# The last two experts' products as three rounded partial products instead of one full float32 product

## What is computed

```python
# attention: 2 batches, 8 heads, 768 positions, head size 64; its output x is (1536, 512)
logits = x @ w_gate                       # 1536 tokens, 8 experts
# tokens go to experts in the order of the sorted logits, 192 tokens each
for e in range(8):
    h = np.maximum(x[mask] @ w1[e], 0.0)  # 192 x 512 by 512 x 1024
    out[mask] = h @ w2[e]                 # 192 x 1024 by 1024 x 512
# dense layer on all rows
h = x @ w_in                              # 512 -> 1024
solu = h * softmax(h)
ln = (solu - mu) / np.sqrt(var + 1e-06) * g_ln
return ln @ w_out                         # 1024 -> 512
```

## Time and profile before

| | |
|---|---|
| median of 3 runs | 492.61 us |
| the profiled execution, its own time | 493.21 us |
| its span | 491.4 us (1.8 us of its time lie outside) |
| PE busy | 473.3 us, 96% of the span |
| DVE, ACT, POOL busy | 341.8, 170.8, 137.3 us |
| chain that ended last | PE 88%, DVE 5%, DMA 2% |
| mean granted TensorE clock | 0.989 of full speed |

### The profile page before, as it was taken

One profiled execution on the slowest core, in us unless ns is written; L12 is line 12 of the kernel. 1 busy time (PEld: TensorE's weight loads), 2 busy tenths in 40 slices (PEclk: granted clock), 3 DMA queues, 4 the chain that ended last, 5 costly groups with the idle time before them and its releaser, 6 DMA issues.

```text
span 491.4 us, 8510 instructions
## 1 busy us (share of the span) xinstructions
PE 473.3 (96%) x3022; PEld 414.4 (84%) x3022; DVE 341.8 (70%) x1108; ACT 170.8 (35%) x354; POOL 137.3 (28%) x213
## 2 busy tenths in 40 slices
PE   7999999999999999999999999999999999999992
PEld 5878878788889899779989988998997899899871
DVE  5777777879888998999789779968966600400451
ACT  3577778723143111433223033322302331220340
POOL 5577877520220300151131112113112141010111
PEclk9899999999999999999999999999999999999996
DMA  8987783110360540092441045045105437000001
GB/s 258 297 257 249 254 260 111 34 33 0 147 229 0 205 171 1 2 336 82 167 167 64 5 176 215 23 169 169 59 5 199 192 119 279 0 23 0 1 21 43
DMA packets 30040, 61.75 MB, mean 126 GB/s; under 512 B 6576, under 2 KB 19760, under 8 KB 25904
## 3 DMA queue, kind: packets, MB, share of 16 engines
q0 software_dynamic: 6592, 39.85, 22.0%
q1 hardware_dynamic: 22544, 20.53, 13.3%
q10 hardware_dynamic: 864, 0.84, 0.6%
HBM read 54.93 MB, written 6.29 MB: 125 GB/s over the span
## 4 chain that ended last, share of the span: by engine, by line
PE 88%; DVE 5%; DMA 2%; issue 1%; ACT 1%; SPq 0%; POOL 0%; DVEq 0%; POOLq 0%
PE psum L1157 17%; PE psum L1174 14%; PE psum L1264 6%; PE psum L1239 5%; PE psum L1246 5%; PE psum L1240 4%; PE psum L1208 4%; PE psum L945 4%; PE psum L1209 4%; PE psum L954 4%; PE psum L1218 4%; PE psum L980 4%; PE psum L977 2%; PE psum L1106 2%; PE psum L1186 2%
## 5 line engine op out<-in xcount | busy, mean ns | idle before, releaser
L1174 PE MATMUL psum<-xs,w_sb 128*128 128x192 f32 x512 | 87.0, 328 | 0.0
L1157 PE MATMUL psum<-shared,w_sb 128*128 128x192 f32 x512 | 84.6, 326 | 0.1
L1157 PEld LDWEIGHTS psum<-shared,w_sb 128*128 128x128 f32 x512 | 83.4, 190 | 1.3 <-issue 0.8
L1174 PEld LDWEIGHTS psum<-xs,w_sb 128*128 128x128 f32 x512 | 83.0, 190 | 0.0
L1546 DVE TENSOR_SCALAR_CACHE_REDUCE key_wide<-keys,thr 128x1536 bf16<-128x1536 f32 x35 | 63.3, 1808 | 0.6
L694 POOL DMA_INDIRECT w_sb<-w,widx x32 | 31.5, 984 | 95.8 <-DVE widx L1639 65.5
L718 POOL TENSOR_TENSOR gain<-spread,cst 128x1 f32<-128x1 f32 x12 | 6.8, 564 | 163.3 <-DVE spread L1701 162.4
L1668 DVE TENSOR_TENSOR yT_lo<-psum,yT_hi 128x384 fp32r<-128x384 f32 x16 | 8.8, 554 | 52.0 <-ACT yT_hi L824 51.8
L1239 PE MATMUL psum<-wout_hi,turned_hi 128*128 128x512 f32 x96 | 38.6, 402 | 1.1 <-ACT turned_hi L824 1.1
L777 ACT ACTIVATE keys<-keys,nmax 128x184 f32<-128x184 f32 x96 | 37.3, 439 | 5.3 <-DVE nmax L1378 5.3
L1208 PE MATMUL psum<-win_hi,yT_hi 128*128 128x512 f32 x96 | 38.5, 401 | 0.0
(11 more groups left out here) (186 smaller groups left out, 848.5 us busy)
## 6 DMA issues: line engine op xcount, KB each, us to landing
shared<-vT SPq DMA_DIRECT2D x8, 384.0 KB, 6.3
shared<-v_main SPq DMA_DIRECT2D x8, 384.0 KB, 3.8
x_rows<-xs SPq DMA_DIRECT2D x8, 384.0 KB, 5.0
shared<-kT SPq DMA_DIRECT2D x7, 384.0 KB, 6.6
shared<-qT SPq DMA_DIRECT2D x7, 384.0 KB, 5.6
w_sb<-w_in SPq DMA_DIRECT2D x4, 512.0 KB, 5.1
w_sb<-w_out SPq DMA_DIRECT2D x8, 256.0 KB, 5.0
w_sb<-v_tail SPq DMA_DIRECT2D x16, 48.0 KB, 3.9
```

What stands on the lines that cost most here:

```text
L1157: mm = pe.matmul(turn[u % 2][:, i * CAP:(i + 1) * CAP], w1_sb[:, par, first:first + P], xT[:, c, :], start=(c == 0), stop=(c == KC - 1))
L1174: mm = pe.matmul(turn[u % 2][:, (d % 2) * CAP:(d % 2 + 1) * CAP], w2_sb[:, par, first:first + P], hT[:, c, :], start=(c == 0), stop=(c == ...
```

## The change

For r = 6 and r = 7 every product of the expert is written as three fp32r products on the same PSUM target, each of 192 columns: high matrix by high tokens, high matrix by low tokens, low matrix by high tokens (`split_products`). The other six experts are as before.

The high part of a matrix is made by ACT as a rounding copy, the low part by DVE as a subtraction, both in four pieces of 128x1024 for each of w1 and w2 (`round_w1`, `round_w2`, `rest_of_w1`, `rest_of_w2`). The low part replaces the matrix in its own buffer, and the high part goes into the buffer of the other parity, the one of expert r - 1. Therefore the gather of w1 for r = 7 now waits for the last hidden unit of r = 6, and that of w2 for the last y of r = 6. Tokens and hidden units are stored rounded by ACT and their rests by DVE (`split_x`, `split_hidden`), in memory of the finished search. `row_numbers(7)` moves to between the hidden and the y products of r = 6; POOL gathers w2 of r = 6 ahead of its tokens; two DVE instructions at the end of the program go.

```diff
+        def rounded(name, shape):
+            return nc.alloc_sbuf_tensor_at(name, shape, F32R, offset=(nc.sbuf_base + 31) // 32 * 32)
...
+        w1_split = rounded("w1_split", [P, 2, KC * FF])
         w1_sb = sb("w1_sb", [P, 2, KC * FF])
+        w2_split = rounded("w2_split", [P, 2, FC * DM])
         w2_sb = sb("w2_sb", [P, 2, FC * DM])
...
             def gather_w1(r):
-                gather_weights(r, w1, w1_sb, in_w1)
+                gather_weights(r, w1, w1_sb, in_w1, hidden_filled[r - 1] if r - 1 in SPLIT else y_filled[r - 2])
             def gather_w2(r):
-                gather_weights(r, w2, w2_sb, in_w2)
+                gather_weights(r, w2, w2_sb, in_w2, y_filled[r - 1] if r - 1 in SPLIT else y_filled[r - 2])
...
+            def round_w1(r, pieces):
+                act.wait_ge(in_w1[r % 2], 32 * (r // 2 + 1))
+                act.wait_ge(unit_filled, hidden_filled[r - 1])
+                for j in pieces:
+                    act.activation(w1_split[:, 1 - r % 2, piece(j)], w1_sb[:, r % 2, piece(j)],
+                                   ACT.Copy).then_inc(w1_hi_ready, 1)
+            def round_w2(r, pieces):
+                act.wait_ge(in_w2[r % 2], 32 * (r // 2 + 1))
+                act.wait_ge(unit_filled, y_filled[r - 1])
+                for j in pieces:
+                    act.activation(w2_split[:, 1 - r % 2, piece(j)], w2_sb[:, r % 2, piece(j)],
+                                   ACT.Copy).then_inc(w2_hi_ready, 1)
...
+                        if ahead:
+                            round_w1(r + 1, range(2))
                         hidden_exp(n)
+                        if ahead:
+                            round_w1(r + 1, range(2, PIECES))
+                        elif r + 1 == SPLIT[0]:
+                            round_w2(r + 1, range(2, 3))
...
+            def split_products(dst, high, low, pair, first, last):
+                pe.matmul(dst, high, pair[:, 0, :], start=first, stop=False)
+                pe.matmul(dst, high, pair[:, 1, :], start=False, stop=False)
+                return pe.matmul(dst, low, pair[:, 0, :], start=False, stop=last)
+            def hidden_split(r, f):
+                par, k = r % 2, SPLIT.index(r)
+                u = at["hidden", r] + f
+                if f == 0:
+                    pe.wait_ge(x_lo_ready, 2 * k + 2)
+                unit_free(u)
+                for i in range(2):
+                    for c in range(KC):
+                        if f == i == 0:
+                            pe.wait_ge(w1_lo_ready, PIECES * k + c + 1)
+                        first = c * FF + (2 * f + i) * P
+                        mm = split_products(turn[u % 2][:, i * CAP:(i + 1) * CAP], w1_split[:, 1 - par, first:first + P],
+                                            w1_split[:, par, first:first + P], x_pair[:, c, :, :], c == 0, c == KC - 1)
+                mm.then_inc(unit_filled, 1)
+            def product_split(r, d):
+                par, k = r % 2, SPLIT.index(r)
+                u = at["y", r, d // 2]
+                if d % 2 == 0:
+                    unit_free(u)
+                for c in range(FC):
+                    if d == 0 and c % 2 == 0:
+                        pe.wait_ge(h_lo_ready, h_unit[at["hidden", r] + c // 2])
+                        pe.wait_ge(w2_lo_ready, PIECES * k + c // 2 + 1)
+                    first = c * DM + d * P
+                    mm = split_products(turn[u % 2][:, (d % 2) * CAP:(d % 2 + 1) * CAP], w2_split[:, 1 - par, first:first + P],
+                                        w2_split[:, par, first:first + P], h_pair(c), c == 0, c == FC - 1)
+                if d % 2:
+                    mm.then_inc(unit_filled, 1)
+            def split_expert(r):
+                for f in range(FC // 2):
+                    hidden_split(r, f)
+                if r == SPLIT[0]:
+                    row_numbers(r + 1)
+                for d in range(KC):
+                    product_split(r, d)
...
-                    if r + 1 == E - 2:
-                        row_numbers(E - 1)
...
+            def split_x(r):
+                for i, (first, n) in enumerate(zip(slots_of(r), (HI, LO))):
+                    u = at["tokens", r] + i
+                    dve.wait_ge(unit_emptied, u + 1)
+                    dve.tensor_tensor(x_pair[:, :, 1, first:first + n],
+                                      turn[u % 2][:, 0:KC * n].rearrange("p (c n) -> p c n", c=KC),
+                                      x_pair[:, :, 0, first:first + n].bitcast(F32), ALU.subtract).then_inc(x_lo_ready, 1)
+            def split_hidden(r, f):
+                u = at["hidden", r] + f
+                dve.wait_ge(unit_emptied, u + 1)
+                dve.scalar_tensor_tensor(h_pairs(f)[:, :, 1, :], turn[u % 2][:, 0:2 * CAP].rearrange("p (c n) -> p c n", c=2), 0.0,
+                                         h_pairs(f)[:, :, 0, :].bitcast(F32), ALU.max, ALU.subtract).then_inc(h_lo_ready, 1)
+            def rest_of_w1(r, pieces):
+                for j in pieces:
+                    dve.wait_ge(w1_hi_ready, PIECES * SPLIT.index(r) + j + 1)
+                    dve.tensor_tensor(w1_split[:, r % 2, piece(j)], w1_sb[:, r % 2, piece(j)],
+                                      w1_split[:, 1 - r % 2, piece(j)].bitcast(F32), ALU.subtract).then_inc(w1_lo_ready, 1)
+            def rest_of_w2(r, pieces):
+                for j in pieces:
+                    dve.wait_ge(w2_hi_ready, PIECES * SPLIT.index(r) + j + 1)
+                    dve.tensor_tensor(w2_split[:, r % 2, piece(j)], w2_sb[:, r % 2, piece(j)],
+                                      w2_split[:, 1 - r % 2, piece(j)].bitcast(F32), ALU.subtract).then_inc(w2_lo_ready, 1)
...
-            link(dve.tensor_scalar(key_wide[:, N // 2:N].bitcast(BF16), hits, 0.5, 0.0, ALU.is_ge, ALU.add,
-                                   accum_out=count[:, :]))
-            link(dve.tensor_scalar(hits, keys[:, :], const("cand0"), None, ALU.is_ge))
```

More of the change, by code:

```diff
@@ L419, in build, with piece @@
         y_unit = {at["y", r, d]: KC // 2 * r + d + 1 for r in range(E) for d in range(KC // 2)}
+        hidden_filled = [at["hidden", r] + FC // 2 for r in range(E)]
+        x_unit = {at["tokens", r] + i: 2 * k + i + 1 for k, r in enumerate(SPLIT) for i in range(2)}
+        h_unit = {at["hidden", r] + f: FC // 2 * k + f + 1 for k, r in enumerate(SPLIT) for f in range(FC // 2)}
+        def piece(j):
+            return slice(j * KC * FF // PIECES, (j + 1) * KC * FF // PIECES)
         norm_unit = {at["norm", n] + c: 2 * n + c + 1 for n in range(ROWS) for c in range(2)}
@@ L890, in _ @@
                 for f in range(FC // 2):
-                    empty_hidden(r, f)
+                    if r in SPLIT:
+                        empty_split_hidden(r, f)
+                    else:
+                        empty_hidden(r, f)
                     if r == 0:
                         add_flags(1, 3 + f)
+                    if r == SPLIT[0] and f == 0:
+                        round_w2(r, range(3, 4))
+                    if r == SPLIT[1] and f < 2:
+                        round_w2(r, range(2 + f, 3 + f))
                 if r == 0:
@@ L903, in _ @@
                     empty_keys(3, range(2, KEY_UNITS))
+                if r == SPLIT[0]:
+                    round_w1(r + 1, range(PIECES))
                 if r == 0:
@@ L906, in _ @@
                 for n in tiles_after(r):
+                    ahead = r + 1 == SPLIT[0] and n == tiles_after(r)[0]
                     if n >= 1:
@@ L917, in _ @@
                         hidden_squares(n)
+                    if ahead:
+                        round_w2(r + 1, range(2))
             empty_turned(ROWS - 1)
@@ new lines, in split_expert, with whole_expert @@
+            def split_expert(r):
+                for f in range(FC // 2):
+                    hidden_split(r, f)
+                if r == SPLIT[0]:
+                    row_numbers(r + 1)
+                for d in range(KC):
+                    product_split(r, d)
+            def whole_expert(r):
+                hidden(r, 0)
+                hidden(r, 1)
+                hidden(r, 2)
+                hidden(r, 3)
+                if r % 2 == 0 and r:
+                    cuts_of(r + 1)
+                product(r, 0)
+                if r % 2 == 0 and r:
+                    ranks_of(r + 1)
+                product(r, 1)
+                if r == 0:
+                    warm(WARM_CUT)
+                    cuts_of(r + 1)
+                if r % 2:
+                    cuts_of(r + 1)
+                if turns_keys(r, 1):
+                    turn_keys(r + 2)
+                product(r, 2)
+                if r % 2 or r == 0:
+                    ranks_of(r + 1)
+                product(r, 3)
@@ L1823, in _ @@
             hidden_gate(m)
+            split_x(SPLIT[0])
+            slots(E - 1)
+            slot_flags(E - 1)
             hidden_spread(m)
-            for r in (E - 2, E - 1):
+            for r in SPLIT:
+                for f in range(FC // 2):
```

(6 more changed lines are left out.)

73 lines of the change are left out of this document (45 added, 28 removed).

## The result

The changed kernel takes 494.86 us (median of 20 runs, 493.12 to 499.50), the kernel before 492.14 beside it: a ratio of 1.0054 (1.0034 to 1.0074). The same kernel run a second time gave 493.48 against 491.98, 1.0034 (1.0020 to 1.0048). So it is slower by a third to a half of a per cent, 1.5 to 2.7 us, just over what can be told from no change. The forecast was 493.8 us.

The account below looks back on a forecast made before the run. PE was taken as the bound, busy 96% of the span. Main term +1.4 us, flags -0.26 and all else hidden gave +1.15 us on the median 492.61, so 493.8 us, range 490.5 to 498.2.

Parts of the forecast that it names:

- The main term: PE, experts 6 and 7: 128 float32 products (41.6 us) become 384 fp32r products at 112 ns (43.0 us), +1.4 us.
- The rule on fast weight load: PE's weight loads: fast for 128 weights unless input is FP32; if on for fp32r, products would be bound by columns.
- Row numbers and flags: 24 small PE products move behind r = 6's hidden products, zero in all; the wait for DVE's flags goes, -0.26 us.
- ACT's pieces: 16 rounding copies at 1.05 us each, hidden ahead of empty_turned for tiles 7 and 8, slacks 0.36 and 0.7 to 1.0.
- the rival: ACT's roundings delay PE at dense_out(7) and dense_out(8): at 1.5 us a piece +1.3 us on top, 495.1 us; chance 0.12.
- DVE's pieces: 16 rests of 128x1024 on DVE at 1.15 us each, all hidden; slack 0.5 us at r = 6's last w2 piece.
- a sign of being wrong: PE waiting over 0.3 us for turned_hi, x_pair, h or w_split, or records 85 to 100 ns apart, would show error.
- The gathers: Loads of w1 and w2 for r = 7, now starting later: both hidden with 2.8 us or more.
- The sum: Whole kernel: +1.4 - 0.26 + 0 = +1.15 us, giving 493.8 us on the median of the runs.
- The columns rival: PE's split products bound by columns at 85 ns: -9.0 - 0.26, 483.3 us; chance 0.13.
- The fixed cost rival: PE's split products carry a fixed cost on top of the load, 123 ns: +5.6 - 0.26, 498.0 us; chance 0.08.
- The clock rival: Clock falls to 1.2 GHz in the split experts, products 160 ns or more: +20.6, 513 us; chance 0.05.

Follow-up runs that it names:

- the moved piece: Changed kernel with the rests of w2 in expert 7 one hidden unit earlier on DVE: 494.23 us, 1.0042 to the kernel before.
- two products: Changed kernel with high matrix by low tokens left out, 256 fp32r products instead of 384: 481.89 us.
- the wide product: Changed kernel with both products of the high matrix made one of 384 columns, halves added afterwards, rests of w2 earlier: 489.35 us, 0.9938 to the kernel before.

## Why the prediction was right, and where it was not

- **The main term** was +1.4 us at 112 ns. It measures 111.4 ns and +1.6: expert 6 +0.84 without the row numbers, expert 7 +0.76 once the wait is taken out. 384 x 0.1114 = 42.8 us are as forecast (43.0). The 0.2 comes of three small things: by PE's starts the four old blocks take 20.67 + 20.66 = 41.33 us and not 4 x 10.40 = 41.6, since the y blocks are a little shorter (10.27) than the hidden ones (+0.3); the pace is 111.4 and not 112 (-0.2); and the y block behind the row numbers takes 0.1 more. Choosing the row nearest to the case, L1239's 0.11 us at a standing start, was right, and the runs show that its reason was, too: half the columns leave 0.11 us as long as the clock is 1.00, half the load brings 90 ns.
- **The rule on fast weight load** (the Trainium skill, TensorE: Matmul & The Clock Gate, Weight-path perf modes) would have had the products bound by columns if fp32r counted as not FP32. Loads are 188 ns long after as well, as in the earlier trace rows, with 111.4 ns between them, against 104 and 32 for bf16: nothing shows it on for fp32r as it is used here, and the profile's rows name the type of these loads f32. The Trainium skill's section LDWEIGHTS on the same page gave an estimate of 107 ns and -0.6 us; the measured pace is 4 ns over it, and with the neutral point at 108 ns these few nanoseconds turn the sign.
- **Row numbers and flags**, forecast 0 and -0.26. The stretch before `hidden(6)` is 0.96 shorter where 1.03 was forecast, and the row numbers come back as 0.85. Together that is -0.11 and not -0.26: of the 0.26 us that stood idle ahead of the row numbers only a part was lost to PE. Its worth was put too low as well: putting both back costs 1.7 us, since the flags' place makes room for DVE's new pieces ahead of the gate, and the row numbers cover the last rest of w2 in expert 6.
- **ACT's pieces**, forecast 1.05 us with slacks of 0.36 and 0.7 to 1.0. Measured 0.97 to 1.06, slacks 0.52 and 1.22. Right, and the rival has no case at this place.
- **DVE's pieces**, forecast 1.15, measured 1.17 to 1.22. Here is the step that failed: "The last w2 piece of r = 6 ends at 408.1 ... Slack 0.5 us. All hidden". It was worked out for r = 6 alone. There the 0.77 us of row numbers stand between the last hidden product and the first y product. For r = 7 nothing stands there, so the same sum gives 0.5 - 0.77 = -0.3, a wait; it measured 0.61, and the moved piece takes it away exactly. The slack of 0.5 us for r = 6 was too large too: without the 0.85 us of row numbers expert 6 lost 0.52, so it was some 0.3. By the prediction's own list a wait of PE for w_split of more than 0.3 us was a sign of being wrong, and this one came.
- **The gathers** were hidden from PE, as forecast; ACT's first rounding of w1 for expert 7 (416.19) has no wait for a DMA ahead of it. For expert 6 the forecast had w1 in 0.9 us ahead of its rounding, and ACT waited 0.69 us for it (374.47), which cost PE nothing.
- **The sum**: +1.15 forecast, +1.89 by stages: +0.61 from the missed wait, +0.2 in the main term, +0.15 in row numbers and flags, and -0.2 in the stretches behind the experts, which no term had. In time it was +1.5 to +2.7. That 493.8 us lies so near the 494.86 and 493.48 is in part luck: it was added to the median of three runs, 492.61, and twenty runs of the kernel before have 492.14. The forecast put it within what can't be told from no change (0.45) and slower at 0.41; it came out slower, just over the line.
- **The columns rival** (85 ns) fell: 111.4. **The fixed cost rival** (123 ns) fell as well, and the argument against it fits: with half the load a product takes 90 ns against 80 of columns, and where the whole load is longer these 10 are not added. **The clock rival** did not come true at 192 columns (1.00 in every stretch), nor with two products; with 96 columns at the same pace it did, at the level of 1.2 GHz that it named, and a product then took 213 ns. So what this rival describes does happen here, but not with the products of this change.

What stays open: why the wide product takes 0.20 us for 384 columns (160 ns by the clock, 170 with the 10 above) while its neighbour takes 0.09. The weight loads of the same execution divide the same 0.287 us otherwise,

```profile
393.88 0.19 PEld L1310 LDWEIGHTS psum<-x_pair,w_split 128*128 128x128 f32 x1
394.06 0.19 PEld L1309 LDWEIGHTS psum<-x_pair,w_split 128*128 128x128 f32 x1
394.16 0.19 PEld L1310 LDWEIGHTS psum<-x_pair,w_split 128*128 128x128 f32 x1
```

0.18 and 0.11, which would suit one load of 111 ns and 176 ns for the 384 columns; nothing here decides it. Open too is where the spread ahead of `hidden(5)` comes from: the lower clock in 12 to 24 us is there in the kernel before, and the 1.2 us of the run with its rests moved earlier came at a granted clock of 1.00. It is as large as the effect.

## What to carry to other kernels

Price a product as the longer of two times, its columns and the load of its stationary operand, each from rows where the other is absent; splitting a float32 product of 128x128 into three fp32r parts gains only where it costs more than three loads of 111 ns, 334 ns, and at 192 columns it costs 325. So put everything with one stationary operand into one product, and count what it costs to add the halves afterwards (1.3 us here). When a slack is worked out for one turn of a loop, work it out for the others: what covers it (here 24 small products) may stand in one turn only. When the effect is under 1%, compare stages from start to start, since spans differ by as much for other reasons.

## What the runs showed of the hardware that was not expected

- A stream of products of 96 columns, 111 ns apart, brought the granted clock from 1.00 to 0.50 within the first expert stage, though PE's row was full, and again within the second, after it had come back between them; with 192 columns at the same pace it stayed at 1.00 for whole stages. At 0.50 the load is 0.33 us long instead of 0.19 and the pace 213 ns instead of 111.4. It is one execution.
- With half the load a product of fp32r takes 10 ns more than its columns (90 for 80 at 192 columns); with the whole load 192 and 96 columns both take 111.4 ns.
- Leaving a third of the products out brought the span from 491.6 to 480.1 us, and halving the columns of all of them raised it to 526.6.
